# Retention and two gated MLPs on one core: operands on one 2 KB grid, identity built on chip, loads and products reordered, fade on ScalarE, last chunk in other banks

## The reference

```
# blocks of 64 tokens; Dmask[i,j] = lam**(i-j) for i >= j, else 0
intra = (q k^T * Dmask) v
inter = (q * lam**(i+1)) kv_state
out   = intra + inter
kv_state = lam**64 * kv_state + (k * lam**(63-i))^T v
```

## Time and profile before

| | |
|---|---|
| Time, median of three | 290.71 us |
| The profiled execution | 289.81 us, of which the span is 287.9 us |
| TensorE busy | 279.2 us, 97% of the span |
| VectorE, ScalarE, GpSimd busy | 58%, 41%, 15% |
| Chain that ended last | TensorE 92%, DMA 4%, VectorE 2%, issue 1% |
| Granted TensorE clock | 1.000 over the span |
| Loads until the attention ends | 250 to 412 GB/s in the first seven slices of 7.2 us |

### The profile page before, as it was taken

How to read it: one execution, slowest core, us unless ns; L and a number is a source line. 1 busy time by engine, 2 the same in 40 slices (tenths; PEclk the granted TensorE clock), 3 DMA queues, 4 the chain that set the end, 5 groups by cost and what they waited for, 6 DMA issues and landing times.

```text
span 287.9 us, 4245 instructions
## 1 busy us (share of the span) xinstructions
PE 279.2 (97%) x1748; PEld 227.0 (79%) x1748; DVE 166.5 (58%) x253; ACT 118.7 (41%) x197; POOL 42.5 (15%) x36
## 2 busy tenths in 40 slices
PE   8799897999999999999999999999999999999996
PEld 8688686888888888888888888888888888888885
DVE  3859998865865103446686644436986499415000
ACT  2027444656784113356822134558215304422121
POOL 0797793007500000000000000000000000000000
PEclk9999999999999999999999999999999999999999
DMA  7999996000000000000000000260000000200212
GB/s 272 412 385 385 393 407 250 0 0 3 0 0 0 0 2 0 0 0 2 0 0 0 3 0 0 61 234 0 0 0 2 0 0 0 112 36 0 109 76 109
DMA packets 7506, 23.42 MB, mean 81 GB/s; under 512 B 832, under 2 KB 1216, under 8 KB 7488
## 3 DMA queue, kind: packets, MB, share of 16 engines
q1 hardware_dynamic: 7344, 23.07, 20.8%
q10 hardware_dynamic: 144, 0.09, 0.1%
HBM read 20.01 MB, written 3.15 MB: 80 GB/s over the span
## 4 chain that ended last, share of the span: by engine, by line
PE 92%; DMA 4%; DVE 2%; issue 1%; ACT 0%; DVEq 0%
PE ps L650 27%; PE ps L652 27%; PE ps L651 27%; PE ps L715 4%; PE ps L666 3%; DMA qk<-in_qk 2%; PE ps L700 2%; PE ps L683 2%; DMA prm<-in_prm 1%; DVE dec L548 1%; DVE qdec L552 1%; DVE pT L462 0%; ACT x L292 0%; ACT out_sb L368 0%; DVE om L554 0%
## 5 line engine op out<-in xcount | busy, mean ns | idle before, releaser
L650 PE MATMUL ps<-xk_h,wk_h 128*128 128x512 f32 x96 | 38.2, 397 | 0.0
L652 PE MATMUL ps<-xk_h,wk_l 128*128 128x512 f32 x96 | 38.1, 396 | 0.0
L652 PE MATMUL ps<-kk_h,wv_l 128*128 128x512 f32 x96 | 38.1, 396 | 0.0
L651 PE MATMUL ps<-kk_l,wv_h 128*128 128x512 f32 x96 | 38.1, 396 | 0.0
L651 PE MATMUL ps<-xk_l,wk_h 128*128 128x512 f32 x96 | 38.1, 396 | 0.0
L650 PE MATMUL ps<-kk_h,wv_h 128*128 128x512 f32 x96 | 38.1, 396 | 0.0
L501 DVE SCALAR_TENSOR_TENSOR kk_f<-ps,ring 128x512 f32<-128x512 f32 x24 | 16.6, 692 | 33.0 <-ACT ring L321 32.8
L525 DVE SCALAR_TENSOR_TENSOR gate<-x,prm,gate 128x512 f32<-128x512 f32 x48 | 32.6, 744 | 0.0
L321 ACT ACTIVATE ring<-ps 128x512 f32<-128x512 f32 x24 | 14.4, 599 | 35.0 <-PE ps L652 35.0
L338 ACT ACTIVATE gate<-x,prm 128x512 f32<-128x512 f32 x12 | 8.7, 725 | 45.1 <-DVE x L511 45.1
L650 PEld LDWEIGHTS ps<-xk_h,wk_h 128*128 128x128 f32 x96 | 18.1, 188 | 4.5 <-issue 0.2
(11 more groups left out here) (69 smaller groups left out, 516.1 us busy)
## 6 DMA issues: line engine op xcount, KB each, us to landing
qk<-in_qk SPq DMA_DIRECT2D x12, 512.0 KB, 5.8
kv<-in_kv SPq DMA_DIRECT2D x12, 512.0 KB, 7.3
out<-out_sb SPq DMA_DIRECT2D x11, 256.0 KB, 2.0
wk_raw<-in_w_k SPq DMA_DIRECT2D x4, 512.0 KB, 7.3
wv_raw<-in_w_v SPq DMA_DIRECT2D x4, 512.0 KB, 9.6
wr_raw<-in_w_r SPq DMA_DIRECT2D x2, 512.0 KB, 8.7
w_raw<-in_w_val SPq DMA_DIRECT2D x2, 512.0 KB, 4.4
w_raw<-in_w_out SPq DMA_DIRECT2D x2, 512.0 KB, 6.9
```

What stands on the lines that cost most here:

```text
L650: nc.tensor.matmul(to, left(0), right(0), start=(i == 0), stop=False)
L651: nc.tensor.matmul(to, left(0), right(1), start=False, stop=False)
L652: done = nc.tensor.matmul(to, left(1), right(0), start=False, stop=(i == last))
```

## The change

- **Memory.** The piece for `x` is rounded up to a multiple of 2 KB, so all that lies behind it is on the grid of the weights.
- **Identity.** It is no longer loaded; `prm` shrinks from 168 to 40 columns. GpSimd makes it with a memset and an affine_select of 128x128.
- **Start.** 8 warming matmuls in place of 12. weigh(0) comes straight behind the 8 scans of dec, ahead of those of qdec. TensorE does scores(0), scores(1), attend(0), update(0), and goes on as before from chunk 1.
- **Loads.** qk of a chunk comes ahead of kv of the chunk before it, and ahead of the weight piece beside it. A load into a used buffer now waits for update as well as attend.
- **Fade.** It moves from GpSimd (one instruction) to ScalarE (four of 128x64, each with its own scale), behind evacuate_x of the chunk before. evacuate_x stands earlier against the work on the weights in some chunks; VectorE's first `low` of w_r moves behind the loop.
- **Last chunk.** inter(11) and attend(11) write banks 0 and 1, so inter(11) waits for weigh(10) and not for the copy of chunk 10. attend(n) waits for the copy only where there is no inter. The banks of all later groups are turned by two.

```diff
-WARM = 12
+WARM = 8
-PRM = IDENT + P
+PRM = CONV + TAPS * KT
-        x_at = take(4 * KT * XW)
+        x_at = take(-(-4 * KT * XW // (2 * KB)) * 2 * KB)
+        def out_banks(n):
+            return (0, 1) if n == NCH - 1 else (4, 5)
-                return (2 * FT * t + n) % 8
+                return (2 * FT * t + n + 2) % 8
...
+            def free(n):
                 if n >= IN_BUFS:
                     sp.wait_ge(att_done, n - IN_BUFS + 1)
+                    sp.wait_ge(update_done, updates(n - IN_BUFS))
+            load_qk(0)
+            load_qk(1)
+            load_kv(0)
+            load_qk(2)
+            load_kv(1)
+            load_qk(3)
+            load_kv(2)
+            load_kv(3)
+            load_qk(4)
             load_weight(wk_raw, w_k, 0, wk_here)
+            load_kv(4)
+            load_qk(5)
             load_weight(wk_raw, w_k, 1, wk_here)
+            load_kv(5)
+            load_qk(6)
+            load_kv(6)
+            load_qk(7)
             load_weight(wk_raw, w_k, 2, wk_here)
+            load_kv(7)
+            load_qk(8)
+            load_kv(8)
+            load_qk(9)
             load_weight(wk_raw, w_k, 3, wk_here)
...
+            nc.gpsimd.memset(ident[:, :], 0.0).then_inc(ident_z, 1)
+            pool.wait_ge(ident_z, 1)
+            nc.gpsimd.affine_select(out=ident[:, :], in_=ident[:, :], compare_op=ALU.not_equal, fill=1.0, base=0,
+                                    pattern=[[-1, P]], channel_multiplier=1).then_inc(ident_ok, 1)
-                fade(n)
...
+            def fade(n):
+                act.wait_ge(state_ready, updates(n - 1))
+                for a in range(PAIRS):
+                    cols = slice(a * D, (a + 1) * D)
+                    nc.scalar.activation(faded[:, cols], state[:, n % 2, cols], ACT.Copy,
+                                         scale=qdec[:, a, CH - 1:CH]).then_inc(faded_ready, 1)
             evacuate_x(0)
+            act.wait_ge(qdec_ok, PAIRS)
+            fade(1)
             evacuate_x(1)
+            fade(2)
             evacuate_x(2)
+            fade(3)
             high(wk, wk_raw, 0, wk_here, wk_hi)
             evacuate_x(3)
+            fade(4)
...
             evacuate_x(8)
+            fade(9)
+            evacuate_x(9)
+            fade(10)
             high(wk, wk_raw, 3, wk_here, wk_hi)
-            evacuate_x(9)
+            evacuate_x(10)
             high(wr, wr_raw, 0, wr_here, wr_hi)
...
+            dve.wait_ge(ident_ok, 1)
             for i in range(H):
...
+            dve.wait_ge(dec_ok, H)
+            weigh(0)
             dve.wait_ge(zero_ok, 1)
             for a in range(PAIRS):
...
-                pe.wait_ge(x_ready, n)
+                if n < NCH - 1:
+                    pe.wait_ge(x_ready, n)
+                else:
+                    pe.wait_ge(p_ready, 2 * n)
...
             scores(0)
-            for n in range(NCH):
+            scores(1)
+            attend(0)
+            update(0)
+            for n in range(1, NCH):
```

More of the change, by code:

```diff
@@ L117, in build @@
         spare = place("spare", [P, 1], own_at + 11 * KB)
+        ident = place("ident", [P, P], own_at + 12 * KB)
         prm = place("prm", [P, PRM], prm_at)
         om = place("om", [P, 2 * KT], prm_at + 4 * PRM)
-        ident = prm[:, IDENT:IDENT + P]
         ps = ctx.enter_context(nc.psum_tensor("ps", [P, 8, 512], F32))
-        ps_s, ps_o, ps_u = [[ps[:, 2 * i + j, :] for j in range(2)] for i in range(2)], [4, 5], [6, 7]
+        ps_s, ps_u = [[ps[:, 2 * i + j, :] for j in range(2)] for i in range(2)], [6, 7]
         f32 = lambda z: z.bitcast(F32)
@@ L235, in _ @@
         def _(pool):
[L236 to L244, removed]
             def decay_k(n):
@@ L374, in _ @@
             evacuate_x(0)
+            act.wait_ge(qdec_ok, PAIRS)
+            fade(1)
             evacuate_x(1)
+            fade(2)
             evacuate_x(2)
+            fade(3)
             high(wk, wk_raw, 0, wk_here, wk_hi)
             evacuate_x(3)
-            for k in range(3):
-                mix_part(0, k, 0)
+            fade(4)
+            mix_part(0, 0, 0)
+            mix_part(0, 1, 0)
             evacuate_x(4)
+            mix_part(0, 2, 0)
             mix_part(0, 3, 0)
             mix_high(0, 0, 0)
-            mix_high(0, 1, 0)
             evacuate_x(5)
             high(wk, wk_raw, 1, wk_here, wk_hi)
+            mix_high(0, 1, 0)
+            evacuate_x(6)
+            fade(7)
             mix_high(0, 2, 0)
             mix_high(0, 3, 0)
-            evacuate_x(6)
             evacuate_x(7)
+            fade(8)
             high(wk, wk_raw, 2, wk_here, wk_hi)
             evacuate_x(8)
+            fade(9)
+            evacuate_x(9)
+            fade(10)
             high(wk, wk_raw, 3, wk_here, wk_hi)
-            evacuate_x(9)
+            evacuate_x(10)
             high(wr, wr_raw, 0, wr_here, wr_hi)
-            evacuate_x(10)
+            evacuate_x(11)
             high(wr, wr_raw, 1, wr_here, wr_hi)
-            evacuate_x(11)
             for k in range(KT):
@@ L546, in _ @@
             dve.wait_ge(prm_here, 16)
+            dve.wait_ge(ident_ok, 1)
             for i in range(H):
-                nc.vector.tensor_tensor_scan(dec[:, i, :], prm[:, LAM_A + i:LAM_A + i + 1].to_broadcast([P, CH]), ident,
-                                             0.0, ALU.mult, ALU.add).then_inc(dec_ok, 1)
+                nc.vector.tensor_tensor_scan(dec[:, i, :], prm[:, LAM_A + i:LAM_A + i + 1].to_broadcast([P, CH]),
+                                             ident[:, :], 0.0, ALU.mult, ALU.add).then_inc(dec_ok, 1)
+            dve.wait_ge(dec_ok, H)
+            weigh(0)
             dve.wait_ge(zero_ok, 1)
@@ L583, in _ @@
                     low(wk, wk_raw, 3, wk_hi, wk_lo)
-                if n == 11:
-                    low(wr, wr_raw, 0, wr_hi, wr_lo)
-            low(wr, wr_raw, 1, wr_hi, wr_lo)
+            for i in range(2):
+                low(wr, wr_raw, i, wr_hi, wr_lo)
             for k in range(KT):
@@ L696, in inter @@
                 pe.wait_ge(state_ready, updates(n - 1))
-                pe.wait_ge(x_ready, n)
+                if n < NCH - 1:
+                    pe.wait_ge(x_ready, n)
+                else:
+                    pe.wait_ge(p_ready, 2 * n)
                 for a in (0, 2, 1, 3):
                     for row in range(2):
-                        last = nc.tensor.matmul(place_of(row, a), state[rows_of(row), n % 2, a * D:(a + 1) * D],
+                        last = nc.tensor.matmul(place_of(n, row, a), state[rows_of(row), n % 2, a * D:(a + 1) * D],
                                                 qd[rows_of(row), inters(n) % 2, a * P:(a + 1) * P],
@@ L709, in attend @@
                 pe.wait_ge(p_ready, 2 * n + 2)
-                if n > 0:
+                if c == 0 and n > 0:
                     pe.wait_ge(x_ready, n)
@@ L714, in attend @@
                         h = head_of(row, a)
-                        last = nc.tensor.matmul(place_of(row, a), kv[i][:, 1, h * D:(h + 1) * D],
+                        last = nc.tensor.matmul(place_of(n, row, a), kv[i][:, 1, h * D:(h + 1) * D],
                                                 pT[:, n % 2, row, a * P:(a + 1) * P],
@@ L725, in hidden @@
                         pe.wait_ge(p_ready, 2 * NCH)
+                if t == 0 and n == 2:
+                    pe.wait_ge(x_ready, NCH - 1)
                 if t == 0 and n == 4:
+                    pe.wait_ge(state_ready, updates(NCH - 1))
+                if t == 0 and n == 6:
                     pe.wait_ge(x_ready, NCH)
-                if t == 0 and n == 6:
-                    pe.wait_ge(state_ready, updates(NCH - 1))
                 if t > 0 and n < KT:
@@ L847 @@
          columns(np.asarray(inputs["moe_mu_k"])), columns(np.asarray(inputs["moe_mu_r"])),
-         columns(np.asarray(inputs["moe2_conv_w"])), np.eye(P, dtype=lam.dtype)], axis=1)
+         columns(np.asarray(inputs["moe2_conv_w"]))], axis=1)
     laid = {
```

44 lines of the change are left out of this document (20 added, 24 removed).

## The result

The changed kernel takes 282.44 us (four runs, 281.16 to 283.30) against 291.08 (290.70 to 291.88): a ratio of 0.9696, with an interval of 0.9652 to 0.9740, that is 8.6 us less where 3.5 were forecast. The profiled execution took 282.59 us with a span of 280.8.

What follows compares the result with a forecast made beforehand. TensorE was taken as the bound: 49 us of attention with loads, then 236 us of matmuls without visible waits. 289.81 - 2.7 (earlier hidden(0,0)) - 0.8 (grid) = 286.3 profiled, median 0.9 above, 287.2; eight-in-ten range 285.7 to 289.4.

Steps and rivals of the forecast that it cites:

- The grid: Big matmuls behind the attention: activations on the weights' grid save 0.00096 us on each of 864, 0.8 us.
- The bounds: Limits of the grid term: gain 0, or a loss of the same size as the 0.8 us.
- The chance that the gain is under 0.9 us: Whole kernel, not below 289.8 us: the same 0.07, slower 0.05, against faster 0.88.
- The start: Up to attend(1): earlier scans and weigh(0) end attend(1) at 14.7 us, not 15.6, a head start of 0.9 us.
- The loads: Waits for qk of chunks 8 and 9: scores(9) at 34.5 us, gain 1.1, bounds 0.5 and 2.2.
- the queue is partly starved, and an earlier attend brings earlier loads: Loads from 14 to 25 us, at 383 GB/s against 419 earlier: scores(8) comes at 31.1 us, gain 0.6.
- The tail: End of the attention: waits ahead of update(10) and inter(11) go, 0.87 and 0.75 us; hidden(0,0) at 46.35.
- The fade on ScalarE: Every chunk: four fades of 0.34 us, 1.35 us (1.1 if neighbours overlap), and nothing waits.
- Free loads: Rival: qk and kv loads on the grid come faster, scores(8) and scores(9) do not wait, 286.1 us; 7%.
- The clock rival: TensorE at the start: fewer warmings and a gap leave chunks at 1.2 GHz, two chunks give 293.8 us; 5%.

Runs made afterwards that it cites:

- e13: The changed kernel with the first w_k piece issued ahead of qk of chunk 4, and 12 warming matmuls, not 8: 281.84 us, ratio 0.9706.
- e5: The changed kernel with activations off the weights' grid by 32 (xk), 64 (xr) and 128 (kk) bytes: 286.15 us.
- e6: The changed kernel with activations off the weights' grid by 256 (xk), 384 (xr) and 512 (kk) bytes: 281.94 us.
- e14: The changed kernel with activations off the weights' grid by 96 (xk), 224 (xr) and 768 (kk) bytes: 284.09 us.
- e7: The changed kernel with the first piece of w_k issued ahead of qk of chunk 4: 279.99 us, ratio 0.9622.
- e10: The changed kernel unaltered, run again beside other load orders: 281.98 us, ratio 0.9682.
- e12: The changed kernel with the first w_k piece issued ahead of qk of chunk 4, and the fade back on GpSimd: 280.30 us, ratio 0.9666.
- e2: The changed kernel with the piece for x back at its old size, activations 160 bytes off again: 288.49 us, ratio 0.9935.
- e1: The kernel before with only the piece for x rounded up to 2 KB: 283.01 us, ratio 0.9736.
- e3: The kernel before with 32 bytes more for x, activations 192 bytes off the weights' grid: 289.25 us.
- e8: The kernel before with x rounded up to 2 KB and the last chunk in banks 0 and 1: 282.57 us, ratio 0.9702.
- e4: The changed kernel with weights and activations all moved up by 32 bytes, distance 0 kept: 280.97 us.

## Why the prediction was wrong

**The step that failed is "The grid".** I read 0.0010 us as the price of the offset from the difference between hidden and project, and took project as the case without a price because its moving operand was on the grid. Its stationary operand was not. What costs is the distance between the two, and both groups had it, 160 bytes one way or the other. The price is 0.0076 us in hidden and 0.0066 in project, so the term is 7.4 us where I put 0.8, and project's matmuls pay too, not the 864 alone. The rows could not give it: no stage of the kernel before had distance 0. The bounds failed with it. They were set at the size of the estimate, and should have asked what remains between 0.2343 us and the 512 columns at 2.4 GHz, 0.2133: 21 us over 1,008 matmuls, all of it open. The chance that the gain is under 0.9 us was put too high for the same reason.

**The start: right.** The scans began at 4.44 (forecast 4.5 to 4.7), identity took 0.29 + 0.20 us on GpSimd by 1.5 us, qdec 1.36 us and clear of kdec(0) (1.3), kdec(1) was the next late thing with TensorE idle 0.99 us ahead of update(1) (0.9), and attend(1) ended at 14.49 (14.7). That the shorter warming gains nothing was wrong (e13). The warming itself took 3.78 us for 16 records and ended at 4.8, not 4.4. And 0.211 us a record is four times, not twice, the 0.053 of 128 columns at 2.4 GHz; that it ran at the lower level is right all the same: in the trace of the kernel before most of its records start 0.213 us apart and the last few 0.112.

**The loads: wrong in the profiled execution, near in others.** scores(9) came at 36.8 and not 34.5, later than the 35.6 of before; in e5, e6 and e14, with the same order of loads, at 34.1 to 34.8. The step "the queue is partly starved, and an earlier attend brings earlier loads" is not borne out: the changed kernel had an earlier attend and a lower rate, with three loads or more always in the queue. I also missed that the change takes one load of nine out of the first batch. It is in the diff: a weight piece behind a load that waits, worth 1.3 to 2 us (e7). GpSimd's kdec waited 8.5 us in all for kv, 2.1 before and 6.1 in e7. In this one execution there was also a break of 1.02 us within scores(4), which waits for nothing the trace shows; it stood at 0.36 in another place of e7 and in none of e10, and its cause is open.

**The tail: half.** The 0.87 us ahead of update(10) went, as forecast: kdec(10) ended at 43.19, 1.3 us before update(10) began. But the fade's move was not needed for it (e12). Of the 0.78 ahead of inter(11), 0.32 came back as a wait for the state, which stands behind VectorE's `low` of 1.79 us. hidden(0,0) was forecast at 46.35; it began at 49.38, and at 46.7 to 49.4 over the seven executions of the table, 47.7 in the middle. Against the 49.0 of the kernel before in that table this is 1.3 us where I put 2.7, and the times of e2 at full clock say the same.

**The fade on ScalarE: right.** 340 ns each and 1.07 us for four, with nothing waiting.

**The rivals.** Free loads did not come: 415 GB/s from 4 to 12 us against 419. The Trainium skill's rule (DMA: Bandwidth & Descriptors, "How a descriptor splits into AXI transactions") was not put to the test: it speaks of where a transaction reads from, the 160 bytes are where the loads write, and the absolute starts are not on record, so it isn't known whether either layout had one on a multiple of 256 bytes. The clock rival is real, but it counts for the change and not against it. In the profiled execution of e1, which has the order of before and 12 warmings, TensorE waited 1.78 us ahead of attend(0), and then (us, busy, clock, DMA share, GB/s):

```profile
10.00:12.00 2.00, 0.82 (x12) 0.89 1.00 399
12.00:14.00 2.00, 2.00 (x18) 0.50 1.05 420
14.00:16.00 2.00, 2.00 (x41) 0.76 0.98 346
```

0.50 is the lower level, 1.2 GHz. The next group of scores took 2.08 us and not 1.16, and hidden began at 50.64. In the profile of e10 the same followed a wait of 1.89 us for loads. The kernel before had the 1.78 us wait too, at a clock of 1.00. So such a wait can cost nothing or some 1.5 us more; I had taken one quiet profile as evidence that it would not happen. Over all executions whose clock is on record, it fell in 21 of the 62 with the start of before (the kernel before, e1, e3, e8) and in 5 of the 46 with the changed start and 8 warming matmuls, 4 of these in the changed kernel and e10. So part of what the medians give to the change is a clock that falls less often. Which edit does that was not tested.

## What to carry to other kernels

Where the time is one long stream of matmuls, work out what each takes beyond its columns at the granted clock before anything else, and treat that whole remainder as open; then put moving and stationary operands at starts a multiple of 256 bytes apart, which cost nothing here and gave 2.6%. When loads are reordered, keep those that wait for nothing ahead of the first one that waits. And read a rate or a wait at the loads from several executions: here one order of loads gave starts of the big products 2.7 us apart, and the one profile of the changed kernel was at the slow end.

## What the runs showed of the hardware that was not expected

- A float32r matmul of 512 columns follows the last after 0.2267 us when the two operands' starts are a multiple of 256 bytes apart, and after 0.2289 to 0.2343 otherwise. Moving both by 32 bytes changed nothing (e4); no other absolute start was tried. For 256 columns the two are nearly the same: 24 of them at the end of project, 0.1200 us apart before, (285.08 - 282.32) / 23, and 0.1197 after.
- The float32 products of the attention did not change with the grid: 1.09, 0.61, 0.60 and 1.02 us a group in both kernels.
- The DMA share hardly tells the rate: from 4 to 12 us before it reads 1.03 with 419 GB/s, from 14 to 25 us after 0.98 with 351.
- TensorE's clock can fall to 1.2 GHz in one execution of a kernel after a wait of 1.8 us, for the stretch shown above, and stay at 2.4 in another.
